# Moving the write and the read of the block inverses in SyncE's queue, and their spreading on ScalarE

## The reference

```python
for t in range(S):
    y[:, :, t] = np.einsum('bhd,bhde->bhe', rt, state)
    Sa = np.einsum('bhde,bhe->bhd', state, at)
    state_decay = state * wt[:, :, None, :] - np.einsum('bhd,bhe->bhde', Sa, bt)
    state = state_decay + np.einsum('bhd,bhe->bhde', vt, kt)
# second layer: h = x @ w_in; h * softmax(h); layer norm; @ w_out
# third layer:  h = x @ w_in; relu(h) + alpha * min(h, 0); @ w_out
```

## Time and profile before

| | |
|---|---|
| median of 3 executions | 1008.28 us (1002.13 to 1009.63) |
| the profiled execution | 1000.47 us, of which its span is 998.7 us |
| TensorE (PE) busy in it | 911.7 us, 91% |
| VectorE (DVE) | 635.8 us, 64% |
| ScalarE (ACT) | 477.5 us, 48% |
| GpSimd (POOL) | 252.4 us, 25% |
| mean share of full clock granted to TensorE | 0.966 |

### The profile page before, as it was taken

The page is one execution under the profiler, slowest core; times in us unless marked ns, Lnnn a source line. Parts: engine busy times, 40 slices in busy tenths (PEclk is TensorE's granted clock), DMA queues, the critical chain, the costliest instruction groups (busy, mean ns, idle before and its releaser), DMA issues.

```text
span 998.7 us, 31704 instructions
## 1 busy us (share of the span) xinstructions
PE 911.7 (91%) x13408; PEld 860.7 (86%) x13408; DVE 635.8 (64%) x1087; ACT 477.5 (48%) x1011; POOL 252.4 (25%) x452
## 2 busy tenths in 40 slices
PE   3379989998798987888999999999999999999998
PEld 2378888988797986777899999999999999999998
DVE  8957766776576754557756656565757565565644
ACT  3336655565454654436534435353535344443533
POOL 9577655775567621000000000000000000000000
PEclk9689989999999999998999999999999999999999
DMA  5635655557465552243010000000000000000000
GB/s 159 134 80 138 160 117 123 143 139 172 92 149 160 122 112 60 84 145 109 14 27 1 27 11 17 27 0 26 0 26 0 26 0 26 0 26 14 1 14 14
DMA packets 144095, 67.35 MB, mean 67 GB/s; under 512 B 118844, under 2 KB 129980, under 8 KB 143980
## 3 DMA queue, kind: packets, MB, share of 16 engines
q1 hardware_dynamic: 143980, 65.66, 26.5%
HBM read 45.98 MB, written 19.66 MB: 66 GB/s over the span
## 4 chain that ended last, share of the span: by engine, by line
PE 51%; POOL 15%; DMA 12%; DVE 8%; issue 6%; SPq 4%; ACT 3%; POOLq 0%; ACTq 0%; DVEq 0%
POOL s_x L831 6%; PE acc L1116 6%; POOL s_t L829 5%; PE acc L1117 5%; PE acc L1118 5%; DMA l_scr<-lb 5%; PE mid L1116 4%; PE mid L1117 4%; PE mid L1118 4%; PE bank L1116 3%; PE bank L1117 3%; PE bank L1118 3%; DMA s_in<-l_scr 3%; DMA d_scr<-s_x 3%; PE bank L1149 2%
## 5 line engine op out<-in xcount | busy, mean ns | idle before, releaser
L1382 POOL TENSOR_TENSOR stats<-stats 128x1 f32<-128x1 f32 x24 | 13.2, 549 | 552.3 <-DVE stats L1444 552.3
L1469 DVE SCALAR_TENSOR_TENSOR stage<-mid,slopes 128x512 f32<-128x512 f32 x96 | 66.3, 691 | 105.2 <-ACT slopes L1310 105.2
L1306 ACT ACTIVATE stage<-mid 128x512 f32<-128x512 f32 x96 | 57.1, 594 | 158.2 <-PE mid L1187 158.2
L1116 PE MATMUL acc<-wo_h,act_h 128*128 128x320 f32 x384 | 121.4, 316 | 6.7 <-DVE act_l L1396 5.9
L1117 PE MATMUL acc<-wo_h,act_l 128*128 128x320 f32 x384 | 118.4, 308 | 0.0
L1118 PE MATMUL acc<-wo_l,act_h 128*128 128x320 f32 x384 | 117.9, 307 | 0.0
L1116 PE MATMUL mid<-zT_h,w_h 128*128 128x256 f32 x384 | 108.0, 281 | 3.2 <-DVE zT_l L1396 3.2
L1117 PE MATMUL mid<-zT_h,w_l 128*128 128x256 f32 x384 | 107.6, 280 | 0.0
L1118 PE MATMUL mid<-zT_l,w_h 128*128 128x256 f32 x384 | 107.4, 280 | 0.0
L808 POOL TENSOR_TENSOR al<-al,prod 40x512 f32<-40x512 f32 x48 | 74.0, 1541 | 93.1 <-DMA al<-a_features_first 77.6
L1310 ACT ACTIVATE slopes<-stage,minus_alpha 128x256 f32<-128x256 f32 x192 | 87.3, 502 | 3.1
(11 more groups left out here) (163 smaller groups left out, 2401.1 us busy)
## 6 DMA issues: line engine op xcount, KB each, us to landing
wkb<-wkb_features_first SPq DMA_DIRECT2D x46, 242.5 KB
rvu<-rv_features_first SPq DMA_DIRECT2D x48, 160.0 KB
l_scr<-lb SPq DMA_DIRECT2D x24, 256.0 KB, 4.4
x_scr<-x SPq DMA_DIRECT2D x24, 256.0 KB, 4.6
al<-a_features_first SPq DMA_DIRECT2D x48, 80.0 KB
sv<-v_time_first SPq DMA_DIRECT2D x48, 80.0 KB, 3.5
out<-y_sb SPq DMA_DIRECT2D x11, 320.0 KB, 2.3
d_scr<-s_x SPq DMA_DIRECT2D x12, 256.0 KB, 2.1
```

The source lines that it names most:

```text
L1116: pe.matmul(o, left[0], right[0], start=start, stop=False)
L1306: act.activation(neg[q % 2][:], mid[q % 2][:], ACT.Relu, scale=-1.0).then_inc(neg_ready, 1)
L1469: dve.scalar_tensor_tensor(out=act_f[q % 2][:], in0=mid[q % 2][:], scalar=0.0, in1=slope[q % 2][:], op0=ALU.max, op1=ALU.add).then_inc(act ...
```

## The change

The write of pair p's inverses leaves SyncE's odd step 2p - 3 and goes into the even step 2p - 2, behind `l_read(p + 1)`; their read goes behind `load_rv` of that step. It holds for p = 2 to 11 (n = 2, 4, ..., 20); pairs 0 and 1 stay in the prologue. On ScalarE, `spread_d` moves behind `take_state` in the same even step. No instruction is added or removed.

```diff
             if n % 2 == 0 and n + 4 < NG:
                 l_read((n + 4) // 2)
+            inverses = n % 2 == 0 and 0 < n < NG - 2
+            if inverses:
+                d_write(n // 2 + 1)
             if n + 8 < NG:
                 load_wkb(n + 8)
             if n > 0:
                 save_y(n - 1)
             if n + 2 < NG:
                 load_rv(n + 2)
-            if n % 2 == 1 and n + 3 < NG:
-                d_write((n + 3) // 2)
+            if inverses:
+                d_read(n // 2 + 1)
             if n + 3 < NG:
                 load_v(n + 3)
-            if n % 2 == 1 and n + 3 < NG:
-                d_read((n + 3) // 2)
...
             if front:
                 spread_a(n + AHEAD)
-            if n % 2 == 0 and n + 2 < NG:
-                spread_d(n // 2 + 1)
             beside(act, n, "mid")
             if 0 < n < NG - 1:
                 take_state(n - 1)
+            if n % 2 == 0 and n + 2 < NG:
+                spread_d(n // 2 + 1)
```

## The result

| | before | after |
|---|---|---|
| median | 1007.69 us (4 executions) | 1062.59 us (4, 1061.14 to 1065.61) |
| profiled execution's span | 998.7 us | 1059.4 us |
| TensorE busy | 911.7 us | 918.4 us |
| mean share of full clock | 0.966 | 0.940 |

The changed kernel takes 1.0558 times as long, with a 95% interval of 1.0508 to 1.0608. Forecast were 1067 us and a range of 1022 to 1100.

The account below looks back on a forecast made before the run. The loop through `l_write`, `l_read`, GpSimd's solve and the inverses' write bounds it at 31 us a pair; nine pairs 347.1 against 280.55, +66.5, less 4, gives +62.5 on 1000.47: 1063, as a median 1067 us; range 1022 to 1100.

Parts of the forecast that it names:

- The mechanism: Even steps: ScalarE's wait for the inverses replaces SyncE's wait for GpSimd's solve; 1067 us, chance 0.72.
- One sign that was named: On SyncE in the changed kernel's profile: it waits for `l_write` to land about 4 us each time.
- S to the start of `l_write`: From TensorE's `solve_u` starting the even step (S) to `l_write`, released by ScalarE's last copy: 0.4 us.
- D: Even step, from the start of `l_write` to the landing of `d_read`: 6.0 + 3.9 + 7.6 = 17.5 us.
- landing of `d_read`: Even step, `d_read` from issue to landing: 4.3 us on a quiet queue plus 3.3 for loads ahead, 7.6.
- spreading to the next step: Even step, from the start of ScalarE's spreading to TensorE's next `solve_u`: 4.7 us.
- The third term: SyncE, `l_read` to the issue of `d_read`: 3.9 us, by the issues ahead or by `d_write`'s landing (3.7 to 4.0).
- The odd step: Step behind TensorE's wait: slow `solve_u` (1.93 us, not 1.13), so 16.7 us each; ends 13.74 and 20.3.
- The end of step 19: ScalarE's 4.00 us wait there for the last write of inverses to land goes away: -4 us.
- The round trip hides: Freed `l_write` breaks the loop, steps run at 13.74 us; D at most 8.8 us; about 971 us, chance 0.07.
- The same mechanism, small: Chain's DMAs overlap the loads fully, TensorE loses nothing at restart: 1005 to 1022 us, about 1015; chance 0.14.
- Much slower: TensorE restarts slowly after each long wait, odd steps like the one of 20.3 us: over 1100 us, chance 0.07.

Follow-up runs that it names:

- SyncE's part alone: The changed kernel with ScalarE's order of before, spreading the inverses ahead of `take_state`: 1070.6 us, 1.0621 times the kernel before.
- the repeated right sides: The changed kernel, with TensorE computing the next step's right side eight times in steps 2, 4, ..., 18: 1042.7 us (seven times, in a second kernel: 1046.7 us).
- the third experiment: The changed kernel with `d_read` directly behind `d_write`, ahead of the loads and the save: 1037.7 us, 1.0297 times the kernel before.
- The last experiment: The changed kernel with the write and read of pair 11's inverses in step 19, as before the change: 1055.6 us, 1.0520 times the kernel before.
- with the inverses first: The changed kernel with the inverses' write heading the even step and their read behind the load of `a`, both ahead of `l_read`: 1001.7 us, 0.9930 times the kernel before.
- the best kernel: The changed kernel with the inverses' write right ahead of `l_write` in the odd step and their read right behind it: 985.3 us, 0.9804 times the kernel before.

## Why the prediction was right, point by point

**The mechanism** held. SyncE's wait for GpSimd disappeared and ScalarE's wait in the even step took its place, along the chain that was named. The experiments back it from three sides: SyncE's part alone does it, the read's place is worth 25 us, and with write and read ahead of `l_read` the whole loss is gone. One sign that was named did not come: SyncE waits for `l_write` to land 1.7 us in the mean (15.7 in 9, 4.0 at most) and not about 4 each time, since it issues the load of `a` meanwhile (2.60 us in step 10); the start of `l_read` is the same by either count.

**The terms**, in the step shown above (251.66 to 274.42) and in the mean of the even steps 2 to 14:

| term | forecast | step 10 | mean |
|---|---|---|---|
| S to the start of `l_write` | 0.4 | 0.3 | 0.3 |
| `l_write` to `l_read` | 6.0 | 5.3 | 5.3 (5.1 to 6.1) |
| `l_read` to the issue of `d_read` | 3.9 | 3.9 | 4.2 (3.6 to 4.6) |
| landing of `d_read` | 7.6 | 8.5 | 7.5 (6.2 to 8.5) |
| D | 17.5 | 17.7 | 17.1 (15.8 to 18.2) |
| spreading to the next step | 4.7 | 4.8 | 4.8 |
| even steps 2 to 14 | 22.6 | 22.8 | 22.2 (20.8 to 23.3) |
| even steps 16 and 18 | 19.3 | | 20.1 |
| odd steps | 16.7 | | 16.2 (14.8 to 17.6) |
| nine pairs, sum | 347.1 | | 341.3 |

`l_read` came a little sooner than the 6.0, near the 5.1 of the other place in the earlier trace rows, and the issue of `d_read` a little later. The errors of D are of both signs and partly cancel. The third term was right by both of its routes at once: in step 10 the issues ahead of `d_read` ended at 261.03 and `d_write` landed at 261.04, and over the nine steps SyncE waited for that landing only 2.1 us in 4 of them. The net of the sum, +62.5 against +60.7 in the profiles, is closer than its terms by luck: the pairs were 5.8 us too high and the end of step 19 too low by 4. The working also adds the medians' offset unevenly, some 4 us for the forecast (1067) and 7 to 8 for the fastest rival (971, where 967 would follow in the same way); nothing hangs on it.

**The odd step.** Its length was right, but its working hides something. The odd steps took 16.2 us, and 15.9 in the mean before; they add 3 us to the difference. The other 58 us are in the even steps, 15.2 in the mean before and 21.7 after. The clock behind the wait costs the changed kernel some 20 us (the gain of the repeated right sides), but the odd steps of the kernel before were nearly as long. The stretches show of what: before, TensorE was busy 133.5 us and idle 9.9 in the nine odd steps, with granted clocks of 0.76 to 0.93 in four of them and full in five; after, it was busy 143.0 and idle 2.9, with 0.81 to 0.88 in all nine. With the repeated right sides the same work takes 121.7 us, at a clock that is full but for one step. So the clock cost about 12 us before and 21 after by that estimate, and the 9.5 us more are largely paid back by 7.0 us less of waiting in the step. The prediction took 16.7 us from one slow step and did not ask of what the 15.9 before were made.

**The end of step 19** was wrong, and it is the one term that failed: "-4" for ScalarE's wait for the last write. That wait did go, since the solve was long done. But from the start of step 20 to the end it takes 621.1 us, and 620.9 before: `d_read(11)` stands behind the save and the load of step 20, and ScalarE waits 4.49 us for it. I had made the sum of what the last pair gains, and not asked of it what I had asked of the other nine. The last experiment gives the gain back: 616.6 us from the start of step 20 to the end.

**The rivals.** *The round trip hides*: out, D was 17.7, not 8.8. *The same mechanism, small*: out; one half of its condition, that the loads ahead of the read cost nothing, is what the third experiment made, and it gave 1037.7 us, not 1015. The other half, that TensorE loses nothing at the restart, is nearly what the repeated right sides made, with 1042.7 us. No run has both; if the two gains of 25 and 20 us added up, it would take an estimated 1018 us. *Much slower*: no odd step took more than 17.6 us. By the fit of the Trainium skill (DMA: Bandwidth & Descriptors, section on the anatomy of one DMA) 256 KB take an estimated 2.6 us. The rows are near that for the write of the inverses on a quiet queue (2.1) and not for their read: 4.25 with no load ahead and 8.51 behind the loads.

## What to carry to other kernels

To take a wait out of a DMA queue, ask not only who stands behind it, but what the waiting item itself will stand behind in its new place, and when its reader wants it. Here `l_write` was freed of the solve altogether in two orders, and that alone was worth little: it cost 55 us where the inverses' read came behind `l_read`, two loads and a save, and gained 5 where write and read stood between `l_write` and `l_read`. The best order leaves `l_write` behind the solve and puts it between the inverses' write and their read, and gains 22 us. In a loop that spans two steps, close the new cycle on paper, and do it for the last round as well, which has other neighbours.

## What the runs showed of the hardware

- How late one and the same write of 256 KB lands depends on what was issued just ahead of it: `d_scr<-s_x` took 2.1 us alone, 3.35 behind the 128 KB of `l_read`, and 5.97 behind the 512 KB of `l_write` (from 194.45, with the inverses first); with `l_write` right behind it, 2.4 in the median.
- SyncE itself is held while it issues the next DMA behind `d_read`, the read of 256 KB in pieces of 64 bytes. In the changed kernel the two v loads there took 7.22 us to issue, where 1.12 is common, and nothing urgent stood behind them. In the kernel before it is a feed-forward weight (3.45 us, where 0.59 is common), and `l_write` of the next pair stands behind it. In the best kernel it is the load of `a` (4.58 us in the step from 220.22). It was longer with the wkb loads ahead (4.8 to 6.8 us for the first v load in steps 2 to 14 of the changed kernel) than without them (3.4 and 3.7 in steps 16 and 18); what holds it, no run shows. The case of step 10:

```profile
261.13 0.80 SPq L229 DMA_DIRECT2D dc<-d_scr  x1
261.98 7.22 SPq L192 DMA_DIRECT2D sv<-v_time_first  x2
```

- More work made a kernel faster: 7 repeated right sides in each of nine steps, some 63 x 1.13 = 71 us of matmuls in otherwise idle time, took 20 us off, since TensorE's clock did not fall.
